# One row of each denominator, laid out by DMA for the reciprocal, and one copy for an even head

## The chip, the cores and the metric

The kernel runs on one core of one Trainium2 chip. The metric is the device time of one execution in microseconds (us). The engines have these names here: TensorE (PE, its weight loads PEld), VectorE (DVE), ScalarE (ACT), GpSimd (POOL) and SyncE (SP), which issues most DMAs.

## What is computed

Three layers follow one another in float32: an attention with a hash mask, a feed-forward layer with the maximum of three products, and one with ELU. The change is in the attention, 16 heads (2 x 8) of 768 positions and 64 columns:

```python
mask = q_bucket[:, :, :, None] == k_bucket[:, :, None, :]
scores = scale * np.matmul(q, k.transpose(0, 1, 3, 2))
scores = np.where(mask, scores, -1000000000.0)
scores = scores - np.max(scores, axis=-1, keepdims=True)
attn = np.exp(scores)
attn = attn / (np.sum(attn, axis=-1, keepdims=True) + 1e-09)
return np.matmul(attn, v).astype(np.float32)
```

The division by the sum of a row is done last, on the outcome of the product with the values.

## The kernel before

The kernel holds its five instruction streams by hand, with semaphores between them. The attention stage runs through slots, from -3 to 18 (`FIRST_SLOT`, `LAST_SLOT`), each of 12 steps; every engine has a function `emit(s)` that is called for each slot and issues in this order whatever that slot has for it. Slot s makes the scores of head s: in each step two products of 128x384 (lines 684, 685) into one of three banks, and ScalarE makes two exponentials of them, `probs` and its rounded `p_hi` (lines 403, 404). GpSimd subtracts the two for `p_lo` (line 336). Six steps later (`LAG`) TensorE multiplies them with the values (lines 699 to 701) into one bank, `pv_ps`. A head has two halves of 384 query positions. Half 0 of head s is finished at the end of slot s, half 1 in the middle of slot s + 1 (line 708 is the last product of either). Meanwhile TensorE multiplies for the row maxima of the next head (line 670, reduced by VectorE at line 540). In odd slots it also transposes the q and k of a coming pair (line 642, at steps 0 and 6, until slot 11), and in even slots it hashes them (lines 654 to 656, at steps 3 and 6, until slot 12).

**The outcome.** `v_hi` has 128 columns: 64 of the head's values and 64 of ones. So the bank has the outcome in partitions 0 to 63 and the denominator of each query in partitions 64 to 127, 64 times the same row. `outcome(s, half)` (line 350), called on ScalarE at steps 0 and 6 ahead of the exponentials, copies both out, each 64x384: the outcome to `x` (line 357), the denominators to `inv` (line 358), in the partitions 0 to 63 for an even head and 64 to 127 for an odd one. A pair of heads fills one unit of 128x384 for each half; four units of `x` and `inv` are in turn. TensorE can start the next half (line 699) when `o_read` says that both copies are done.

**The division.** VectorE takes the reciprocal of a whole unit in two parts of 128x192 (`reciprocals`, line 592), one ahead of maximum 9 of slot u + 2 (`INV_AT`) and one at its end, and multiplies (`divide`, line 587) at the end of that slot. ScalarE rounds the unit to `xh` (line 442) at step 3 of slot u + 3 and GpSimd makes `xl` (line 342) from the rest. The first products of the feed-forward layer read `xh` and `xl`: `piece` in slots 15 and 16 and the experts behind slot 16. A barrier of all engines stands between the attention and the rest.

**SyncE's queue.** In each slot it loads the values of the next head (line 256, behind `vl_done` and `vsum_done`). In even slots it loads the next q and k (`load_qk`, line 230), and then spreads the hashed pair: operands (lines 239, 280), and the bits behind a wait for `bits_done` (line 293). Ahead of slot 12's spread it loads six weight tiles (line 262). Odd slots have nothing but the load of the values, so that the queue runs ahead into the next even slot. In slot 14 ScalarE rounds a weight tile of 128x1536 at step 9 (line 428).

Of the kernel before, what the change touches and what calls it, by code (L numbers as in the profile page):

```python
# [28 lines left out]
FP32 = mybir.dt.float32  # L29
# [8 lines left out]
HEADS = B * H  # L38
# [30 lines left out]
INV_AT = 9  # L69
V_AT, X_AT = 0, 3  # L70
EMPTY_AT = 4


class Slot:
# [17 lines left out]
    has_unit = property(lambda s: 0 <= s.off - 2 < HEADS)  # L92
    has_split = property(lambda s: 0 <= s.off - 3 < HEADS)
    has_tp = property(lambda s: s.odd and -3 <= s.off < HEADS - 3)
# [9 lines left out]
def wait(eng, sem, count):  # L104

    if count > 0:
        eng.wait_ge(sem, count)


def attention(nc, q, k, v, proj, w1, w2, w3, xh, xl, raw, wh, wl, banks, w_loaded, w_split, w_ready, f_ready):  # L110
    ctx = ExitStack()
    with ctx:
# [3 lines left out]
        def sem(name):  # L116
            return ctx.enter_context(nc.semaphore(name))
# [47 lines left out]
        inv = sb("inv", [P, 4, HALF])  # L165

        st_ps = [banks[:, i, :] for i in range(RING)]
        mx_ps = [banks[:, RING + i, :] for i in range(2)]
# [42 lines left out]
        o_read = sem("o_read")  # L211
        inv_done = sem("inv_done")
        x_done = sem("x_done")
        xh_done = sem("xh_done")
# [9 lines left out]
        def _(sp):  # L224
# [23 lines left out]
            load_qk(1, 1, 0)  # L248

            def emit(s):  # L250
                if s.has_max:
# [7 lines left out]
                if s.off == HEADS - 4:  # L259
                    for m in range(2):  # L260
                        for j, w in enumerate((w1, w2, w3)):
                            sp.dma_start(raw[:, m, j * DM:(j + 1) * DM].rearrange("p (t n) -> p t n", n=P),
                                         w[:, m * P:(m + 1) * P].rearrange("(t p) n -> p t n", p=P)
                                         ).then_inc(w_loaded[m], 16)
                if not s.odd and 0 <= s.off < HEADS - 4:

                    load_qk(s.count(0.5, 2), s.off // 2 % 2, s.count(1, 2))
                if s.has_hash:
# [18 lines left out]
                    if s.off == FIRST_SLOT + 3:  # L287
                        sp.wait_ge(consts, 14)
                    both = s.count(1, 4)
                    sp.wait_ge(bits_done, both)  # L290
# [9 lines left out]
        def _(pool):  # L300
# [29 lines left out]
            def emit(s):  # L330
                for step in range(STEPS):
                    if s.has_st:

                        pool.wait_ge(exp_done, s.count(STEPS, step + 1))
                        at = (STEPS * s.off + step) % KEPT
                        pool.tensor_tensor(p_lo[:, at, :], probs[:, step % RING, :], p_hi[:, at, :].bitcast(FP32),  # L336
                                           ALU.subtract).then_inc(pl_done, 1)
                    if s.has_split and step == X_AT:

                        pool.wait_ge(xh_done, s.count(1, -2))  # L340
                        out = bass.ds(s.count(HALF, -3 * HALF), HALF)
                        pool.tensor_tensor(xl[:, out], x[:, (s.off - 3) % 4, :], xh[:, out].bitcast(FP32),
                                           ALU.subtract).then_inc(xl_done, 1)
# [4 lines left out]
        def _(act):  # L348

            def outcome(s, half):  # L350

                h = s.off - 1
                rows, unit = slice(h % 2 * D, h % 2 * D + D), h // 2 * 2 % 4 + half
                if h % 2 == 0 and half == 0:
                    wait(act, xl_done, s.count(1, -3))
                act.wait_ge(pv_ready, s.count(2, half - 1))
                act.activation(x[rows, unit, :], pv_ps[0:D, 0:HALF], ACT.Copy).then_inc(o_read, 1)
                act.activation(inv[rows, unit, :], pv_ps[D:P, 0:HALF], ACT.Copy).then_inc(o_read, 1)  # L358
# [29 lines left out]
            def emit(s):  # L388
                for step in range(STEPS):
# [39 lines left out]
                    if s.has_st and step == EMPTY_AT:  # L429
# [3 lines left out]
                        if s.off == 0:  # L433
# [5 lines left out]
                                       ).then_inc(empty_done, 1)  # L439
                    if s.has_split and step == X_AT:  # L440
                        act.wait_ge(x_done, s.count(1, -2))
                        act.activation(xh[:, bass.ds(s.count(HALF, -3 * HALF), HALF)], x[:, (s.off - 3) % 4, :],
                                       ACT.Copy).then_inc(xh_done, 1)

# [3 lines left out]
        def _(dve):  # L448
# [67 lines left out]
            def emit(s):  # L516
                m = s.off + 1
                for n in range(STEPS):
# [4 lines left out]
                    if n == MAX_BEFORE[V_AT + 2] and s.has_st:  # L523
# [3 lines left out]
                                          v_hi[:, par, :, 0:D].bitcast(FP32), ALU.subtract).then_inc(vl_done, 1)  # L527
                    if n == INV_AT and s.has_unit:
                        reciprocals(s, 1)

                    if n == MAX_BEFORE[TP_AT[0] + 3] and s.has_tp and s.off != FIRST_SLOT + 2:
# [10 lines left out]
                if s.has_max:  # L542
# [3 lines left out]
                                      ).then_inc(max_done, 1)  # L546
                if s.has_unit:
                    reciprocals(s, 0)
# [26 lines left out]
                if s.has_max:  # L575
                    value_sum(s)
                if s.has_unit:
                    divide(s)
                if s.off == HEADS - 2:
# [6 lines left out]

            def divide(s):
                dve.wait_ge(inv_done, s.count(2, -2))
                unit = (s.off - 2) % 4
                dve.tensor_tensor(x[:, unit, :], x[:, unit, :], inv[:, unit, :], ALU.mult).then_inc(x_done, 1)  # L590
# [606 lines left out]
```

## Time and profile before

| | |
|---|---|
| median of three runs | 746.25 us (744.72 to 748.39) |
| the profiled execution | 746.78 us, span 745.0 us |
| TensorE (PE) busy | 721.2 us, 97% of the span |
| ScalarE (ACT) busy | 423.2 us, 57% |
| VectorE (DVE) busy | 383.4 us, 51% |
| GpSimd (POOL) busy | 369.5 us, 50% |
| line 540, maxima, DVE x192 | 99.5 us, 548 ns each |
| lines 403 and 404, exponentials, ACT x384 | 190.1 us, 495 ns each |
| line 336, p_lo, POOL x192 | 198.8 us, 1053 ns each |

The attention stage is the part up to about 297 us. In the page's forty slices of 18.6 us the three other engines are at 7 to 9 tenths there and TensorE at 9:

```profile
PE   6899999999999999999999999999999999999998
...
DVE  6768988989888863322222211244344333444333
ACT  4388989989899882131222121265556555555553
POOL 5277889888888882011110010254544445454442
```

Each digit is the busy share of a slice in tenths. A matmul is pipelined, and its record is longer than the distance to the next one's start; so a TensorE that is shown as busy can still lose time between two starts, which the timeline shows.

### The profile page before, as it was taken

The numbers are of one execution on the slowest core, as the hardware profiler recorded it, in microseconds if no ns is written. First come the engines' busy times: TensorE is split into PE (matmuls) and PEld (weight loads), VectorE is DVE, ScalarE is ACT, GpSimd is POOL, SyncE is SP. The second block draws the span as 40 slices with busy tenths as digits, with TensorE's granted clock in tenths as the row PEclk, the third lists the DMA queues.
The fourth block names the chain that finished last, engine by engine and source line by source line (L and its number), as shares of the span: only waits on it lengthen the run. The fifth ranks groups of instructions, "written<-read, shape, count | busy, mean of one in ns | idle before, by whom it ended". The sixth has DMA issues, their size and how long they took to land.

```text
span 745.0 us, 9831 instructions
## 1 busy us (share of the span) xinstructions
PE 721.2 (97%) x3469; PEld 619.2 (83%) x3469; DVE 383.4 (51%) x616; ACT 423.2 (57%) x820; POOL 369.5 (50%) x333
## 2 busy tenths in 40 slices
PE   6899999999999999999999999999999999999998
PEld 5699998999998877788888888878888888888886
DVE  6768988989888863322222211244344333444333
ACT  4388989989899882131222121265556555555553
POOL 5277889888888882011110010254544445454442
PEclk8799999999999999999999999999999999999999
DMA  7655366563673000311000001133334333443231
GB/s 148 139 129 131 83 134 137 115 131 79 135 181 72 1 0 1 86 42 43 22 21 1 22 22 43 45 103 108 86 111 144 100 98 90 109 141 109 90 99 57
DMA packets 79321, 63.50 MB, mean 85 GB/s; under 512 B 29080, under 2 KB 68712, under 8 KB 79272
## 3 DMA queue, kind: packets, MB, share of 16 engines
q1 hardware_dynamic: 77416, 62.47, 32.8%
q10 hardware_dynamic: 1856, 0.40, 0.3%
q8 instruction: 28, 0.46, 0.3%
q14 instruction: 21, 0.17, 0.1%
HBM read 40.91 MB, written 3.15 MB: 59 GB/s over the span
## 4 chain that ended last, share of the span: by engine, by line
PE 59%; DVE 0%; ACT 0%; issue 0%; DVEq 0%
PE banks L786 14%; PE banks L788 14%; PE banks L787 14%; PE banks L1142 6%; PE banks L1138 6%; PE banks L1139 6%; DVE g_sb L1081 0%; DVE g_sb L1077 0%; DVE e L1061 0%; DVE e L1057 0%; DVE out_sb L1051 0%; ACT gh L1036 0%; ACT neg L1031 0%; ACT e L1008 0%; DVEq L1060 0%
## 5 line engine op out<-in xcount | busy, mean ns | idle before, releaser
L948 POOL TENSOR_TENSOR wl<-raw,wh 128x512 fp32r<-128x512 f32 (+2 forms) x104 | 143.5, 1398 | 296.8 <-ACT wh L964 296.8
L336 POOL TENSOR_TENSOR p_lo<-probs,p_hi 128x384 fp32r<-128x384 f32 x192 | 198.8, 1053 | 55.2 <-ACT p_hi L404 54.3
L786 PE MATMUL banks<-xh,wh 128*128 128x512 f32 x408 | 159.1, 390 | 2.8 <-DVE e L1061 2.6
L787 PE MATMUL banks<-xl,wh 128*128 128x512 f32 x408 | 158.8, 389 | 0.0
L788 PE MATMUL banks<-xh,wl 128*128 128x512 f32 x408 | 158.8, 389 | 0.0
L540 DVE TENSOR_REDUCE half_max<-banks 128x1 f32<-128x384 f32 x192 | 99.5, 548 | 29.0 <-PE banks L670 28.0
L403 ACT ACTIVATE probs<-banks 128x384 f32<-128x384 f32 x192 | 95.0, 495 | 29.2 <-PE banks L685 23.9
L404 ACT ACTIVATE p_hi<-banks 128x384 fp32r<-128x384 f32 x192 | 95.1, 495 | 0.0
L1077 DVE TENSOR_SCALAR g_sb<-banks 128x512 f32<-128x512 f32 x48 | 33.2, 692 | 119.8 <-ACT neg L1031 119.8
L786 PEld LDWEIGHTS banks<-xh,wh 128*128 128x128 f32 x408 | 76.6, 188 | 19.3 <-issue 3.0
L788 PEld LDWEIGHTS banks<-xh,wl 128*128 128x128 f32 x408 | 76.6, 188 | 16.0
L787 PEld LDWEIGHTS banks<-xl,wh 128*128 128x128 f32 x408 | 76.6, 188 | 15.4
L1138 PE MATMUL banks<-wh,gh 128*128 128x512 f32 x192 | 74.9, 390 | 0.2 <-ACT gh L1036 0.2
L1142 PE MATMUL banks<-wh,gl 128*128 128x512 f32 x192 | 74.9, 390 | 0.0
L1139 PE MATMUL banks<-wl,gh 128*128 128x512 f32 x192 | 74.7, 389 | 0.0
L699 PE MATMUL banks<-p_hi,v_hi 128*128 128x384 f32 x192 | 66.8, 348 | 5.9 <-ACT inv L358 5.5
L1031 ACT ACTIVATE neg<-banks 128x512 f32<-128x512 f32 x48 | 28.7, 598 | 68.5 <-PE banks L788 68.5
L964 ACT ACTIVATE wh<-raw 128x512 fp32r<-128x512 f32 (+2 forms) x104 | 64.6, 665 | 2.3
L701 PE MATMUL banks<-p_hi,v_lo 128*64 128x384 f32 x192 | 65.2, 339 | 0.0
L700 PE MATMUL banks<-p_lo,v_hi 128*128 128x384 f32 x192 | 64.4, 335 | 0.0
L1010 ACT ACTIVATE hh<-e 128x512 fp32r<-128x512 f32 x18 | 11.4, 632 | 92.2 <-DVE e L1061 92.2
L1036 ACT ACTIVATE gh<-g_sb 128x512 fp32r<-128x512 f32 x48 | 30.4, 633 | 40.8 <-DVE g_sb L1081 40.8
(121 smaller groups left out, 1191.9 us busy)
## 6 DMA issues: line engine op xcount, KB each, us to landing
operands<-wh SPq DMA_DIRECT2D x36, 384.0 KB, 7.0
raw<-in_moe_w_in SPq DMA_DIRECT2D x48, 256.0 KB, 2.7
raw<-in_moe_w_out SPq DMA_DIRECT2D x48, 256.0 KB, 2.7
raw<-in_moe_w SPq DMA_DIRECT2D x18, 256.0 KB, 3.8
wl<-wh SPq DMA_DIRECT2D x9, 384.0 KB, 6.4
v_raw<-in_v SPq DMA_DIRECT2D x16, 192.0 KB, 2.5
out_dram<-out_sb SPq DMA_DIRECT2D x12, 256.0 KB, 2.1
q_raw<-in_q SPq DMA_DIRECT2D x15, 192.0 KB, 3.6
```

What stands on the lines that cost most here:

```text
L336: pool.tensor_tensor(p_lo[:, at, :], probs[:, step % RING, :], p_hi[:, at, :].bitcast(FP32), ALU.subtract).then_inc(pl_done, 1)
L403: act.activation(probs[:, step % RING, :], scores, ACT.Exp, scale=SCALE)
L404: act.activation(p_hi[:, (STEPS * s.off + step) % KEPT, :], scores, ACT.Exp, scale=SCALE).then_inc(exp_done, 1)
L540: dve.tensor_reduce(half_max[:, m % 2, n // 2, n % 2:n % 2 + 1], bank[:, 0:HALF], AX.X, ALU.max).then_inc(mx_read, 1)
L699: pe.matmul(out, v_hi[:, h % 2, kt, :], p_hi[:, kept, :], start=(kt == 0), stop=False)
L786: pe.matmul(out, sh, mh, start=first, stop=False)
L787: pe.matmul(out, sh, ml, start=False, stop=False)
L788: last = pe.matmul(out, sl, mh, start=False, stop=final)
L948: pool.tensor_tensor(wl[:, j, at:at + cols], raw[:, j, at:at + cols], wh[:, j, at:at + cols].bitcast(FP32), ALU.subtract).then_inc(w_ready, 1)
L1138: pe.matmul(acc[t], gh[:, n % 2, cols], w2h, start=(k == 0), stop=False)
L1139: pe.matmul(acc[t], gh[:, n % 2, cols], w2l, start=False, stop=False)
L1142: last = pe.matmul(acc[t], gl[:, n % 2, cols], w2h, start=False, stop=(k == M2 - 1))
```

## The change

Heads 14 and 15 stay as they are. For heads 0 to 13:

- An even head's outcome and denominators are copied from the bank to `x` in one instruction of 128 partitions, 64 of which the odd head overwrites later. An odd head's are copied in two: the outcome (64x384) as before, and one row of denominators (1x384) to row 64 of `inv`.
- When both halves of a head are out, SyncE gathers its row of 768 denominators into 12 rows of 64 (`rec`, `gather`). ScalarE waits for the even head's gather before it overwrites the rows.
- VectorE takes one reciprocal of 24x64 for each pair (`compact_recips`), ahead of maximum 2 of odd slots. SyncE writes it to DRAM, waits, and broadcasts each head's row of 768 to 64 partitions of `inv` (`spread_recips`).
- The products follow one slot later for the first unit of a pair: both wait for the broadcasts, one at the end of an odd slot, one ahead of maximum 3 of the even slot behind it. The splits into `xh` and `xl` of a pair are both in the even slot, at steps 3 and 9 (3 and 4 in slot 16), and none in odd slots up to 15.

```diff
@@ SyncE
+            def gather(s):
+                h, u = s.off - 1, (s.off - 1) // 2 * 2 % 4
+                a, par = h % 2, h // 2 % 2
+                sp.wait_ge(o_read, s.count(4))
+                sp.dma_start(rec[a * PIECES:(a + 1) * PIECES, par, :], (inv if a else x)[D:D + 1, u:u + 2, :]
+                             ).then_inc(den_in[a], 16)
+            def spread_recips(s):
+                g = (s.off - 3) // 2
+                par, u = g % 2, 2 * g % 4
+                sp.wait_ge(rec_done, g + 1)
+                sp.dma_start(rec_rows[par], rec[:, par, :]).then_inc(rec_out, 16)
+                sp.wait_ge(rec_out, 16 * (g + 1))
+                for a in range(2):
+                    row = rec_rows[par][a * PIECES:(a + 1) * PIECES].rearrange("c n -> (c n)")
+                    sp.dma_start(inv[a * D:(a + 1) * D, u:u + 2, :].rearrange("p a n -> p (a n)"),
+                                 row.unsqueeze(0).to_broadcast([D, S])).then_inc(inv_in, 16)
...
+                if s.has_recip:
+                    spread_recips(s)
+                if s.has_gather and not s.has_hash:
+                    gather(s)
                 if not s.odd and 0 <= s.off < HEADS - 4:
                     load_qk(s.count(0.5, 2), s.off // 2 % 2, s.count(1, 2))
...
+                    if s.has_gather:
+                        gather(s)
                     both = s.count(1, 4)
                     sp.wait_ge(bits_done, both)
@@ ScalarE, outcome
-                if h % 2 == 0 and half == 0:
-                    wait(act, xl_done, s.count(1, -3))
+                if h % 2 == 0:
+                    wait(act, xl_done, s.count(1, half - 4))
                 act.wait_ge(pv_ready, s.count(2, half - 1))
+                if h < HEADS - 2 and h % 2 == 0:
+                    act.activation(x[:, unit, :], pv_ps[:, 0:HALF], ACT.Copy).then_inc(o_read, 2)
+                    return
+                if h < HEADS - 2:
+                    act.wait_ge(den_in[0], 8 * s.off)
+                    act.activation(x[rows, unit, :], pv_ps[0:D, 0:HALF], ACT.Copy).then_inc(o_read, 1)
+                    act.activation(inv[D:D + 1, unit, :], pv_ps[D:D + 1, 0:HALF], ACT.Copy).then_inc(o_read, 1)
+                    return
@@ ScalarE and GpSimd, the splits
+SPLIT_AT = {(HEADS + 1, 3): HEADS - 2, (HEADS + 2, 3): HEADS - 1}
+for g in range(PAIRS - 1):
+    SPLIT_AT[2 * g + 4, 3] = 2 * g
+    SPLIT_AT[2 * g + 4, 9 if 2 * g + 4 < HEADS else 4] = 2 * g + 1
@@ VectorE
-                    if n == INV_AT and s.has_unit:
+                    if n == INV_AT and s.is_direct:
                         reciprocals(s, 1)
+                    if n == 2 and s.has_recip:
+                        compact_recips(s)
+                    if n == 3 and not s.odd and 4 <= s.off <= HEADS:
+                        wait_spread(s)
+                        divide(s.off - 3)
...
-                if s.has_unit:
-                    divide(s)
+                if s.has_recip:
+                    wait_spread(s)
+                    divide(s.off - 3)
+                if s.is_direct:
+                    dve.wait_ge(inv_done, 2 * (s.off - HEADS + 1))
+                    divide(s.off - 2)
...
+            def compact_recips(s):
+                g = (s.off - 3) // 2
+                for a in range(2):
+                    dve.wait_ge(den_in[a], 16 * (g + 1))
+                dve.reciprocal(rec[:, g % 2, :], rec[:, g % 2, :]).then_inc(rec_done, 1)
+            def wait_spread(s):
+                dve.wait_ge(inv_in, 32 * ((s.off - 3) // 2 + 1))
```

`is_direct` holds in slots 16 and 17, `has_gather` in slots 1 to 14, and `has_recip` in the odd slots 3 to 15.

## Rows read from the trace of the kernel before

**Rows 1.** Waits over the whole span: engine line <- awaited: us total, times, longest.
```profile
PEld banks L699 <- ACT inv L358: 11.7, 18, 1.3
...
PE banks L699 <- ACT inv L358: 5.5, 13, 1.0
```

**Rows 2.** Windows: stretch, length, busy time (x instructions) per engine, PEclk, DMA share, GB/s.
```profile
137.90:153.00 15.10, 15.00 (x91) 14.09 (x90) 13.43 (x23) 14.81 (x35) 13.18 (x14) 1.00 0.36 80
122.00:137.90 15.90, 15.58 (x90) 14.58 (x89) 13.92 (x25) 13.79 (x31) 13.17 (x14) 1.00 0.72 158
```

**Rows 3.** Timeline of PE, 145 to 155: start, length, line, operation [idle before].
```profile
145.50 0.34 PE L708 MATMUL banks<-empty,total 128*128 128x384 f32 x1
...
147.22 0.34 PE L685 MATMUL banks<-operands 128*128 128x384 f32 x1
147.66 0.45 PE L699 MATMUL banks<-p_hi,v_hi 128*128 128x384 f32 x1
147.94 0.34 PE L700 MATMUL banks<-p_lo,v_hi 128*128 128x384 f32 x1
148.11 0.34 PE L701 MATMUL banks<-p_hi,v_lo 128*64 128x384 f32 x1
...
154.54 0.44 PE L699 MATMUL banks<-p_hi,v_hi 128*128 128x384 f32 x1 [0.31 <-ACT inv L358]
```

**Rows 4.** Timeline of ACT in the same stretch.
```profile
144.90 0.94 ACT L436 ACTIVATE empty<-operands,below_one 12x768 fp32r<-12x768 f32 x1
...
146.61 0.48 ACT L357 ACTIVATE x<-banks 64x384 f32<-64x384 f32 x1
147.12 0.49 ACT L358 ACTIVATE inv<-banks 64x384 f32<-64x384 f32 x1
```

**Rows 5.** Groups by line, VectorE's reciprocals: busy us, mean ns, idle before.
```profile
L597 DVE RECIPROCAL inv<-inv 128x192 f32<-128x192 f32 x32 | 42.6, 1339 | 9.5 <-ACT inv L358 9.5
```

**Rows 6.** Timeline of ACT, then PE, where slot 6 becomes slot 7.
```profile
137.02 0.49 ACT L404 ACTIVATE p_hi<-banks 128x384 fp32r<-128x384 f32 x1
...
137.93 0.34 PE L684 MATMUL banks<-operands 128*128 128x384 f32 x1
```

**Rows 7.** Timeline of PE in slots 13 to 15, one window, timeline of ACT.
```profile
232.68 0.44 PE L699 MATMUL banks<-p_hi,v_hi 128*128 128x384 f32 x1 [0.18 <-ACT inv L358]
...
240.71 0.44 PE L699 MATMUL banks<-p_hi,v_hi 128*128 128x384 f32 x1 [0.68 <-ACT inv L358]
...
263.73 0.44 PE L699 MATMUL banks<-p_hi,v_hi 128*128 128x384 f32 x1 [1.01 <-ACT inv L358]
...
264.00:268.00 4.00, 4.00 (x16) 3.72 (x16) 2.98 (x3) 3.03 (x9) 4.00 (x5) 0.58 0.00 0
...
251.54 0.53 ACT L442 ACTIVATE xh<-x 128x384 fp32r<-128x384 f32 x1
251.95 0.49 ACT L403 ACTIVATE probs<-banks 128x384 f32<-128x384 f32 x1
...
259.81 1.49 ACT L428 ACTIVATE wh<-raw 128x1536 fp32r<-128x1536 f32 x1
```

**Rows 8.** Timeline of SyncE's DMA issues (merged where xN, N over 1).
```profile
142.08 1.31 SPq L230 DMA_DIRECT2D q_raw<-in_q  x2
...
153.12 1.17 SPq L280 DMA_DIRECT2D operands<-wh  x2
...
204.31 4.17 SPq L262 DMA_DIRECT2D raw<-in_moe_w  x6
```

**Rows 9.** Timeline of DVE, the product at the end of slot 7.
```profile
153.73 0.55 DVE L590 TENSOR_TENSOR x<-x,inv 128x384 f32<-128x384 f32 x1
```

**Rows 10.** DMA issues by line: count, KB each, median us from issue to landing.
```profile
operands<-wh SPq DMA_DIRECT2D x36, 384.0 KB, 7.0
...
v_raw<-in_v SPq DMA_DIRECT2D x16, 192.0 KB, 2.5
...
proj_raw<-in_proj SPq DMA_DIRECT2D x2, 3.0 KB, 4.4
```

More of the change, by code:

```diff
@@ L69 @@
 INV_AT = 9
-V_AT, X_AT = 0, 3
+V_AT = 0
+PIECE = 64
+PIECES = S // PIECE
+SPLIT_AT = {(HEADS + 1, 3): HEADS - 2, (HEADS + 2, 3): HEADS - 1}
+for g in range(PAIRS - 1):
+    SPLIT_AT[2 * g + 4, 3] = 2 * g
+    SPLIT_AT[2 * g + 4, 9 if 2 * g + 4 < HEADS else 4] = 2 * g + 1
 EMPTY_AT = 4
@@ L92 @@
     has_unit = property(lambda s: 0 <= s.off - 2 < HEADS)
-    has_split = property(lambda s: 0 <= s.off - 3 < HEADS)
+    is_direct = property(lambda s: s.has_unit and s.off >= HEADS)
+    has_gather = property(lambda s: 0 <= s.off - 1 < HEADS - 2)
+    has_recip = property(lambda s: s.odd and 3 <= s.off < HEADS)
     has_tp = property(lambda s: s.odd and -3 <= s.off < HEADS - 3)
@@ L165, in attention @@
         inv = sb("inv", [P, 4, HALF])
+        rec = sb("rec", [2 * PIECES, 2, PIECE])
+        rec_rows = nc.dram_tensor("rec_rows", (2, 2 * PIECES, PIECE), FP32, kind="Internal").ap()
         st_ps = [banks[:, i, :] for i in range(RING)]
@@ L212, in attention @@
         inv_done = sem("inv_done")
+        den_in = [sem(f"den_in{a}") for a in range(2)]
+        rec_done = sem("rec_done")
+        rec_out = sem("rec_out")
+        inv_in = sem("inv_in")
         x_done = sem("x_done")
@@ L337, in emit @@
                                            ALU.subtract).then_inc(pl_done, 1)
[L338 to L342, printed above, removed]
+                    if (s.off, step) in SPLIT_AT:
+                        u = SPLIT_AT[s.off, step]
+                        pool.wait_ge(xh_done, u + 1)
+                        out = slice(u * HALF, (u + 1) * HALF)
+                        pool.tensor_tensor(xl[:, out], x[:, u % 4, :], xh[:, out].bitcast(FP32),
                                            ALU.subtract).then_inc(xl_done, 1)
@@ L439, in emit @@
                                        ).then_inc(empty_done, 1)
[L440 to L443, printed above, removed]
+                    if (s.off, step) in SPLIT_AT:
+                        u = SPLIT_AT[s.off, step]
+                        act.wait_ge(x_done, u + 1)
+                        act.activation(xh[:, u * HALF:(u + 1) * HALF], x[:, u % 4, :], ACT.Copy).then_inc(xh_done, 1)
             all_slots(emit)
@@ L576, in emit @@
                     value_sum(s)
-                if s.has_unit:
-                    divide(s)
+                if s.has_recip:
+                    wait_spread(s)
+                    divide(s.off - 3)
+                if s.is_direct:
+                    dve.wait_ge(inv_done, 2 * (s.off - HEADS + 1))
+                    divide(s.off - 2)
                 if s.off == HEADS - 2:
@@ L585, in emit, with divide @@
                                       ).then_inc(w_ready, 1)
-            def divide(s):
-                dve.wait_ge(inv_done, s.count(2, -2))
-                unit = (s.off - 2) % 4
+            def compact_recips(s):
[5 more added lines that the diff above has]
+                dve.wait_ge(inv_in, 32 * ((s.off - 3) // 2 + 1))
+            def divide(u):
+                unit = u % 4
                 dve.tensor_tensor(x[:, unit, :], x[:, unit, :], inv[:, unit, :], ALU.mult).then_inc(x_done, 1)
```

## The prediction

> **What bounds the kernel now.** I read the idle times of the waits view first, then the windows, then the timelines of each engine over two slots. In the attention stage (about 40 to 297 us) TensorE is busy nearly all the time, at the full granted clock: 15.00 of 15.10 us in slot 7 (odd) and 15.58 of 15.90 us in slot 6 (even) [rows 2]. VectorE, at 13.43 and 13.92 us, has a tenth to an eighth of each slot free. So work taken from VectorE is worth nothing unless somebody waits for it. The one wait of TensorE that comes back every slot is line 699, the first product with the values after a half is finished: it waits for ScalarE's second copy out of the bank (line 358), 13 times as idle of the matmuls and 18 times as idle of the weight loads [rows 1]. What those stalls cost is read from starts. Two matmuls of 384 columns start 0.17 to 0.175 us apart (147.94, 148.11) although each record is 0.34 long. Between 147.22 and 147.66 lie 0.44 us, so 0.26 are lost though the row names no idle, and the stalled matmul itself is followed 0.28 instead of 0.17 later: another 0.11 [rows 3]. Where the row shows idle, the loss is that idle plus 0.17, which the record of the matmul before hides, plus the same 0.11: 0.31 in the row at 154.54 is a loss of 0.59 in all.
>
> Why the wait is there differs by slot. In slot 7 the half ends at 145.84, but ScalarE comes to the copies only at 146.61: it has worked without a pause since the slot began (14.81 of 15.10 us), with the empty-row product of 0.94 just before, and two copies in a row then keep the bank until 147.61 [rows 2 to 4]. At the start of an even slot ScalarE is on time, and the two copies (1.0 us) are simply longer than the matmuls in between.
>
> **What the change does to TensorE's stalls.** Heads 0 to 12, the even ones, get one copy of 128 partitions instead of two of 64. The price of one copy goes by the columns: 0.48 for 64x384 and 0.49 for the 128x384 of line 403 [rows 4, 7], so I take 0.49 and the bank is free 0.5 us sooner. Odd slots also lose the split of line 442, 0.41 us from start to the next start [rows 7], and so ScalarE is no longer 0.75 late at 146.61. The even heads' stalls lie in the middle of odd slots and at the start of odd slots (covered by the six transposes there, except in slot 13, which has none).
> Gains: slots 3, 5, 7, 9 and 11, five stalls like that of slot 7, from 0.26 to 0.33 plus about 0.11: 5 x 0.39 = 1.95. Slot 1, where ScalarE has no backlog: 0.22. Slot 13, middle: idle 0.68, loss 0.68 + 0.17 + 0.11 = 0.96. Slot 13, start: idle 0.18, loss 0.46 [rows 7]. Sum 3.6 us. That is the ceiling: the odd heads (stalls of 0.59 at the start of slots 2, 4 and so on, and the middle of slot 14) keep two copies, since a copy of one row has as many columns as one of 64 rows. Between nothing (0.1) and the nearest row (0.49) for the one-row copy I take 0.49; the low end would give 7 x 0.4 = 2.8 us more, and I leave a part of that in the range.
> Costs: the split moves into step 9 of even slots. ScalarE's pass of step 10 of slot 6 ends at 137.51 and the scores of slot 7 that need it start at 137.93: 0.42 of room [rows 6] for an insertion of 0.41. So between 0 and 0.1 in each of slots 4, 6, 8 and 10; I take 0.05, 0.2 in all. In slot 12 nothing covers the next copy, so 0.37 of the 0.46 above comes back. In slot 14 the split stands right behind the 1.49 us of line 428, ahead of the worst stall of the stage (idle 1.01, at 263.73) [rows 7], and goes on top of it: 0.41 to 0.53, I take 0.45. Net: 3.6 - 0.2 - 0.37 - 0.45 = 2.6 us.
>
> **VectorE and the reciprocals.** Heads 0 to 13 lose 28 reciprocals of 1.339 us, 37.5 us of busy time [rows 5], and get 7 of 24x64. If the price follows the columns each is 1.339 x 64/192 = 0.45; the bounds are nothing and the 1.34 of the whole part. Nobody on TensorE's path waits for them: I cost the saving at nothing. What hides the new compact one is VectorE's free time, over 1 us a slot [rows 2].
>
> **SyncE and the DMAs.** New in every slot is a gather (3 KB, 12 rows of 256 B), issued once both halves of a head are out, at mid-slot; in odd slots also one write of 6 KB to DRAM, a wait for it, and two broadcasts of 192 KB. Prices by the nearest rows: a small strided load lands 4.4 us after its issue, 192 KB after 2.5, and 384 KB in a busy queue after 7.0 [rows 10]. Behind the odd slots' gather SyncE now holds the next v load and the four q/k loads. They go out from 142.08 now [rows 8], and at about 147 to 151 after. They land by about 153, just as the operands' spread begins (153.12 [rows 8]), and are read a slot later. Before slot 12 the six weight loads (204.31, 1.5 MB) go out near 210 and run some 2 us into the spread of slot 12; the hash rows behind it have 1 to 2 us of room. I cost both at nothing; with the cover gone it is 1 to 2 us once.
> ScalarE waits for the even head's gather before it overwrites the rows: issued about 146.5, landed at 151 by the slow price and needed once slot 7's last half is out, just after 153. VectorE waits at the third maximum of odd slots for a gather issued 6 us before, and at the end of odd slots for the broadcasts: with slot 7 starting at 137.9 and three maxima ahead of the end of the reciprocal, I put its end at about 141; the write is issued and landed by 141 + 0.65 + 2.5 (or 4.4), broadcasts issued in 1.3, landed 2.5 (or 4.4) later: 148 (or 152). The product starts at 153.73 [rows 9], the latest moment at which the broadcasts cost nothing. It holds, with 2 to 6 us to spare.
> The Trainium skill (DMA: Bandwidth & Descriptors, "Anatomy of one DMA — SWDGE (gpsimd) path") speaks against this route: about 2 us fixed for each transfer, most of it the receipt of the last byte, "surprisingly long" when the target is HBM. With two transfers in series that is 4 us and the data's time, and the broadcasts would still be there before the product, so the sum would be the same; only its "surprisingly long" would be rival (c), below.
>
> **Tail.** Heads 14 and 15 keep the old way. The stage ends with TensorE's products of the first experts, and units 14 and 15 keep their times, so nothing is gained or lost there.
>
> **The sum.** The profiled execution took 746.78 us (span 745.0, 1.8 outside). 746.78 - 2.6 = 744.2. It lies 0.5 over the median of 746.25, from which the same gain gives 743.7: that is the forecast, 0.35% faster. A difference under about 0.5% can hardly be told from none for this kernel, and so "no difference" is the likeliest verdict.
>
> **Rivals.**
> (a) A new wait takes the stall's place: ScalarE's extra split at step 9 costs TensorE 0.4 in each even slot (its room is only 0.42), and the stall in odd slots ends in a wait for the scores. Gain 3.6 - 4 x 0.4 (slots 4, 6, 8, 10) - 0.8 (slots 12 and 14) = 1.2: 745.1. For it: the room of 0.01. Against: ScalarE is idle for 15.90 - 13.79 = 2.1 us of slot 6 [rows 2].
> (b) The clock. After the stall at 263.73 the granted clock falls to the 1.2 GHz level (mean 0.58 over 264 to 268) [rows 7]: 4 x 0.42 x 2 = 3.4 us at half speed, worth up to 1.7 us. If the shift of a few us moves this away, the time is 743.7 - 1.5 = 742.2; the longer stall in slot 14 speaks rather for a drop that stays. The Trainium skill (TensorE: Matmul & The Clock Gate, "Part 1: The HAM clock gate (the "warmup" mystery)") has the clock released by activity, which the fall behind the idle agrees with.
> (c) Slower: the way through DRAM. It decides when the broadcasts land after the end of the odd slot. If the two broadcasts, 64 reads of one row each, take the 7.0 us of the busy queue and the write 4.4, they land at 141 + 0.65 + 4.4 + 1.3 + 7.0 = 154.4, 0.7 too late, and the maxima behind the product keep TensorE waiting. From there every us more costs 7 us, once for each of the seven pairs. 2 us late: 743.7 + 14 = 758. Against: the queues are nearly empty then (mean DMA share 0.36) [rows 2].
> (d) The one-row copy is cheap or odd slots' lower load helps elsewhere: 741.5.
>
> **Chances.** Forecast 0.48 (own range 742.6 to 745.2), (a) 0.20, (b) 0.12, (c) 0.12, (d) 0.08. Faster by over 0.5% (below 742.5): (b), (d) and a little of the forecast, 0.24. Slower by over 0.5% (above 750): (c), 0.12. Within: 0.64. The range leaves out most of (c) and the far end of (d): 741.0 to 747.5.
>
> **What would show it.** In the profile after: line 699's idle after the copy gone in the middle of odd slots, left at 0.31 at the start of even ones; slots 3 to 11 shorter in pairs by 0.4 us; the compact reciprocal near 0.45; VectorE's idle up by some 30 us with no gain from it; the stall near 262 longer by 0.4. The prediction is wrong if VectorE waits for DMAs at the compact reciprocal or the product, if line 670 waits for the hash rows at slot 13, or if a pair of slots gains over 1 us.

## The result

The changed kernel takes 753.06 us (median of five runs, 751.29 to 755.02) against 746.25 before: a ratio of 1.0091, 95% interval 1.0072 to 1.011. It is 6.8 us slower, where 2.6 us less were forecast, and outside the range of 741.0 to 747.5. The profiled execution took 755.02 us, with a span of 753.2.

The page after: first the busy times, then the slices of TensorE and VectorE.

```profile
span 753.2 us, 9862 instructions
...
PE 722.1 (96%) x3469; PEld 618.2 (82%) x3469; DVE 358.2 (48%) x595; ACT 416.7 (55%) x806; POOL 371.2 (49%) x333
...
PE   7899999999999889899999999999999999999998
...
DVE  6757777777786654322222221143434343443333
```

VectorE has 25 us less to do (383.4 before), TensorE the same (721.2 before). The slices of the attention show TensorE at 8 here and there where it had 9. The windows of slots 6 and 7, which answer to [rows 2] (stretch, length, busy time by engine, granted clock, DMA share, GB/s):

```profile
122.40:139.80 17.40, 15.99 (x92) 14.82 (x90) 13.21 (x23) 13.96 (x33) 13.58 (x14) 1.00 0.73 156
139.80:154.60 14.80, 14.80 (x90) 13.96 (x90) 10.97 (x21) 13.76 (x32) 13.13 (x14) 1.00 0.37 93
```

The odd slot behaves as forecast: 14.80 us long instead of 15.10, TensorE busy to the last tenth. The even slot has grown from 15.90 to 17.40, and TensorE is idle for 1.4 us of it. The waits of the attention stage say for whom (answering [rows 1]; us in total, times, longest):

```profile
PEld banks L743 <- DVE half_max L599: 13.7, 17, 1.4
...
PE banks L743 <- DVE half_max L599: 8.2, 10, 1.1
...
PE banks L772 <- ACT inv L409: 2.9, 8, 0.8
PE banks L772 <- ACT inv L412: 2.7, 3, 1.3
```

The wait for ScalarE's copies: the matmuls' idle for it is 2.9 us at line 409, the odd heads' second copy, and 2.7 at line 412, that of heads 14 and 15, which keep the old copies; none is listed for the even heads' single copy (line 403), whose one stall, in the middle of slot 13, is a loss of 0.39 us read from starts. In its place stands line 743, the product for the row maxima, which waits for VectorE (line 599), 8.2 us in ten waits of the matmuls and more of the weight loads. In the waits view of the kernel before that wait was 1.4 us in all. The timeline of TensorE in slot 6 (start, length, line, idle before) shows one of them:

```profile
126.70 0.34 PE L758 MATMUL banks<-operands 128*128 128x384 f32 x1
128.13 0.44 PE L743 MATMUL banks<-operands 96*128 96x384 f32 x1 [1.09 <-DVE half_max L599]
128.41 0.34 PE L727 MATMUL banks<-wh,proj_hi 128*128 128x384 f32 x1
```

From 126.70 to 128.13 are 1.43 us for a distance of 0.17: 1.26 lost, and 0.11 more behind. VectorE's timeline of the same moment:

```profile
124.97 0.56 DVE L599 TENSOR_REDUCE half_max<-banks 128x1 f32<-128x384 f32 x1 [0.42 <-PE banks L743]
125.45 0.86 DVE L580 TENSOR_TENSOR v_lo<-v_raw,v_hi 128x384 fp32r<-128x384 f32 x1
126.24 1.38 DVE L663 TENSOR_TENSOR x<-x,inv 128x384 f32<-128x384 f32 x1
127.54 1.63 DVE L599 TENSOR_REDUCE half_max<-banks 128x1 f32<-128x384 f32 x3
```

Behind maximum 2 (124.97) stand the values' low part, 0.86 us, and then the moved product `x * inv`, 1.38 us. Only at 127.54 do the next maxima follow. The maxima have two banks between TensorE and VectorE (`mx_ps` in the kernel), and TensorE stops once both wait to be read: here 2.0 us lie between VectorE's maxima (125.53 to 127.54).

The lengths of the slots in TensorE's timelines, in us. A slot is measured from start to start of the last product of half 0 (line 708 before, 781 after), and its first half ends where the last product of half 1 starts:

| slot | before | changed | e1, product at 9 | e4, one copy alone | e6, e4 with GpSimd free |
|---|---|---|---|---|---|
| 5, first half | 7.69 | 7.90 | 7.89 | 8.25 | 7.70 |
| 5, second half | 7.38 | 6.94 | 6.95 | 6.94 | 6.95 |
| 6 | 16.06 | 17.36 | 16.05 | 16.05 | 16.04 |
| 12 | 16.05 | 17.34 | 16.03 | 16.04 | 16.02 |
| 13 | 14.76 | 14.61 | 15.91 | 14.17 | 14.18 |
| 14 | 15.04 | 16.27 | 15.03 | 15.06 | 15.05 |
| 15 | 20.00 | 20.46 | 20.44 | 20.02 | 20.03 |

Slots 7, 9 and 11 are like 5, and 4, 8 and 10 like 6, within 0.06 us. The sum over slots 3 to 14 of "changed" less "before": five even slots 6.52, slot 14 1.23, four odd ones -0.89, slot 3 +0.09, slot 13 -0.15. That is +6.8 us, as much as the medians differ. The two profiled executions are 8.2 us apart; the other 1.4 lie outside these slots, where the granted clock falls at different places. One of these places hides a further cost of the change in slot 15, which is taken up behind e9.

### The profile page after: what moved, and what is told of

It is laid out like the page before. It is cut to its first block, busy times and chain, and to the rows that moved or that the text cites. A ratio compares the mean times of both kernels' runs of the same rounds, so it can differ in the third digit from the quotient of the medians.

```text
span 753.2 us, 9862 instructions
## 1 busy us (share of the span) xinstructions
PE 722.1 (96%) x3469; PEld 618.2 (82%) x3469; DVE 358.2 (48%) x595; ACT 416.7 (55%) x806; POOL 371.2 (49%) x333
## 4 chain that ended last, share of the span: by engine, by line
PE 59%; DVE 0%; ACT 0%; issue 0%; DVEq 0%
PE banks L859 14%; PE banks L860 14%; PE banks L861 14%; PE banks L1211 6%; PE banks L1215 6%; PE banks L1212 6%; DVE g_sb L1154 0%; DVE g_sb L1150 0%; DVE e L1134 0%; DVE e L1130 0%; DVE out_sb L1124 0%; ACT gh L1109 0%; ACT neg L1104 0%; ACT e L1081 0%; DVEq L1133 0%
## 5 line engine op out<-in xcount | busy, mean ns | idle before, releaser
L743 PE MATMUL banks<-operands 96*128 96x384 f32 x144 | 43.7, 354 | 10.2 <-DVE half_max L599 7.9
```

## Experiments

Theory A: VectorE's crowd ahead of maximum 3 of the even slots costs the time. Rival B: the new way of the denominators through DMA and DRAM does.

**e1_product_at_9.** The even slots' product of the changed kernel goes ahead of maximum 9, where the kernel before has a reciprocal.

```diff
-                    if n == 3 and not s.odd and 4 <= s.off <= HEADS:
+                    if n == (9 if s.off < HEADS else 3) and not s.odd and 4 <= s.off <= HEADS:
                         wait_spread(s)
                         divide(s.off - 3)
```

> The changed kernel with one edit: in even slots 4 to 14 the product of a pair's second unit stands ahead of maximum 9 on VectorE instead of ahead of maximum 3, where the low part of the values (0.86 us) stands too. Theory A (VectorE's crowd ahead of maximum 3): in the changed kernel TensorE loses 1.26 + 0.12 us at line 743 in each even slot from 4 to 14, waiting for the maximum behind the two operations. With the product at 9 these go, even slots are 16.0 us instead of 17.35, and the time falls by about 6 x 1.3 = 8 us, to 745, near the kernel before. Rival B (the way through DRAM, or the DMAs added, hold the even slots): the product only waits elsewhere, and the time stays within 2 us of 753.

Measured: 746.98 us, 1.0017 of the kernel before (1.0004 to 1.0029). Slot 6 is 16.05 us again. In the slots the line gives back what theory A expected, 7.8 us over the six even slots, but slot 13 gets 1.3 us longer. So the median comes back by 6.1 us, where 8 were expected. VectorE's timeline in slot 6 of this kernel:

```profile
123.75 0.86 DVE L580 TENSOR_TENSOR v_lo<-v_raw,v_hi 128x384 fp32r<-128x384 f32 x1
124.54 1.64 DVE L599 TENSOR_REDUCE half_max<-banks 128x1 f32<-128x384 f32 x3
...
129.72 0.55 DVE L663 TENSOR_TENSOR x<-x,inv 128x384 f32<-128x384 f32 x1
```

The maxima follow the low part at once (124.54), and the same product takes 0.55 us at its new place instead of 1.38. That difference is taken up behind e6.

The medians leave 1.0 us over the kernel before. Against that kernel, slot 13 has 1.15 us too much (15.91 instead of 14.76) and slot 15 0.4, while slots 5, 7, 9 and 11 are 0.9 us shorter together. TensorE's timeline in slot 13, and SyncE's issues before it:

```profile
229.56 0.34 PE L758 MATMUL banks<-operands 128*128 128x384 f32 x1
231.37 0.62 PE L743 MATMUL banks<-operands 96*128 96x384 f32 x2 [1.47 <-DMA operands<-bits]
...
209.15 3.68 SPq L299 DMA_DIRECT2D raw<-in_moe_w  x6
213.26 1.41 SPq L321 DMA_DIRECT2D operands<-wh  x2
214.71 6.07 SPq L256 DMA_DIRECT2D operands<-wh  x4
```

TensorE waits 1.47 us for the hash rows. The six weight loads went out at 209.15 instead of 204.31 [rows 8], the spread of the operands right behind them from 213.26. In the changed kernel itself this stall is almost hidden (a loss of 0.25 us); its slot 12 is 1.3 us longer, which gives the transfers that time.

**e2_before_extra_product.** The other way round: the kernel before with one more product ahead of maximum 3 in slots 4, 6 to 14.

```diff
+                    if n == 3 and not s.odd and 4 <= s.off < HEADS:
+                        dve.wait_ge(x_done, s.off - 2)
+                        dve.tensor_tensor(scratch[:], x[:, (s.off - 3) % 4, :], inv[:, (s.off - 3) % 4, :], ALU.mult).then_inc(extra, 1)
```

> The kernel before with nothing of the change but one added operation: in even slots 4 to 14 VectorE multiplies a unit once more into a tile that nobody reads, ahead of maximum 3, where the changed kernel has its moved product. Theory A: 6 stalls of about 1.3 us at line 670, +7 to +8 us, 1.010 of the kernel before. Rival B: VectorE has room for it, under +1.5 us.

Measured: 753.62 us, 1.0105 (1.009 to 1.012). Its waits show the changed kernel's wait, with almost its sum (8.2):

```profile
PE banks L675 <- DVE half_max L545: 7.9, 8, 1.1
```

The even slots 4 to 12 are 17.35 us long, slot 14 16.28. One operation at that place makes the loss, without anything else of the change.

**e3_after_no_route.** The changed kernel without `gather`, `spread_recips` and the three waits for them; inv and rec are filled with ones at the start.

> The changed kernel without the way of the denominators: no gather, no write to DRAM, no broadcast, and none of the waits for them; it leaves out that part of the computation (the division is by ones laid down at the start, and by the rows that the copies leave). All operations of the engines stay. Theory A: the time stays at 752 to 753, the stall at line 743 in even slots stays at 1.1 us of idle. Rival B: it falls by 6 to 9 us. A third possibility, that the later loads of q, k and the weights cost something once or twice, would show as 0.5 to 2 us.

Measured: 753.25 us, 1.0104 (1.0085 to 1.0123), the changed kernel's time. The wait stays:

```profile
PE banks L739 <- DVE half_max L594: 8.4, 11, 1.1
```

Rival B falls: the route costs nothing that the time shows. The rows of the changed kernel say why: landing of the broadcasts (count, KB, us from issue), the issues of slot 7, and the two small operations.

```profile
inv<-rec_rows SPq DMA_DIRECT2D x14, 192.0 KB, 3.3
...
142.03 0.33 SPq L280 DMA_DIRECT2D rec_rows<-rec  x1
143.33 1.16 SPq L284 DMA_DIRECT2D inv<-rec_rows  x2
149.02 0.82 SPq L272 DMA_DIRECT2D rec<-x  x1
...
L655 DVE RECIPROCAL rec<-rec 24x64 f32<-24x64 f32 x7 | 3.7, 530 | 0.0
...
L409 ACT ACTIVATE inv<-banks 1x384 f32<-1x384 f32 x14 | 6.7, 482 | 0.3
```

The broadcasts go out at 143.33 and land 3.3 us after their issue, long before the product at the end of the slot; and the wait for the write takes 1.3 us with its issue (142.03 to 143.33), with SyncE's next issue only at 149.02.

**e4_before_one_copy.** The kernel before with the one copy of the even heads and nothing else but a tile of ones for the reciprocals.

```diff
+                if h < HEADS - 2 and h % 2 == 0:
+                    act.wait_ge(inv_set, 1)
+                    act.activation(x[:, unit, :], pv_ps[:, 0:HALF], ACT.Copy).then_inc(o_read, 2)
+                    return
```

> The kernel before with only the one copy of 128 partitions for the even heads 0 to 12; it leaves out that their denominators reach the tile of the reciprocals (they divide by ones laid down at the start). The reciprocals, the products and the splits are where they were. By the prediction's sum this is worth 2.8 to 3.6 us (the stalls of TensorE in the middle of odd slots and at slot 13), ratio 0.995 to 0.996. If the stalls only move (its rival a), the gain is under 1 us.

Measured: 745.55 us, 0.9989 (0.9976 to 1.0003): no gain that can be told from none, where the sum had promised 2.8 to 3.6 us. The table shows where it went. The second half of odd slots gained what was forecast (7.38 to 6.94), but their first half went from 7.69 to 8.25. The kernel before, VectorE (the low part of the values, maxima) and GpSimd at the start of slot 7:

```profile
141.01 0.66 DVE L526 TENSOR_TENSOR v_lo<-v_raw,v_hi 128x384 fp32r<-128x384 f32 x1
...
136.71 3.27 POOL L336 TENSOR_TENSOR p_lo<-probs,p_hi 128x384 fp32r<-128x384 f32 x3 [0.18 <-ACT p_hi L404]
140.24 1.01 POOL L336 TENSOR_TENSOR p_lo<-probs,p_hi 128x384 fp32r<-128x384 f32 x1 [0.26 <-ACT p_hi L404]
141.55 1.01 POOL L336 TENSOR_TENSOR p_lo<-probs,p_hi 128x384 fp32r<-128x384 f32 x1 [0.29 <-ACT p_hi L404]
```

and e4_before_one_copy, the same stretch, with TensorE's stall at the end:

```profile
141.07 1.34 DVE L531 TENSOR_TENSOR v_lo<-v_raw,v_hi 128x384 fp32r<-128x384 f32 x1
142.34 1.01 DVE L545 TENSOR_REDUCE half_max<-banks 128x1 f32<-128x384 f32 x2
...
136.77 5.23 POOL L337 TENSOR_TENSOR p_lo<-probs,p_hi 128x384 fp32r<-128x384 f32 x5 [0.19 <-ACT p_hi L409]
...
142.36 0.34 PE L691 MATMUL banks<-operands 128*128 128x384 f32 x1
142.94 0.44 PE L676 MATMUL banks<-wl 96*128 96x384 f32 x1 [0.23 <-DVE half_max L545]
```

Before, GpSimd has subtracted all that it had by 139.98, does one from 140.24 to 141.25, and has nothing until 141.55. VectorE's low part starts at 141.01, with 0.24 us of that subtraction left, and ends 0.42 us behind it: 0.66 us. In e4_before_one_copy ScalarE is through with the copy half a microsecond sooner and begins its exponentials sooner, and GpSimd has five subtractions without a pause up to 142.00. The low part starts at 141.07, 0.09 us behind the start of the last of them, and ends 0.41 us behind its end: 1.34 us. The maxima behind it are late, and TensorE loses 0.40 us at line 676 (142.36 to 142.94). By these rows the copy's shorter time has closed a pause of GpSimd that VectorE lived on. So theory C: VectorE's operations with two operands in SBUF wait for GpSimd's running one.

Slot 13, for which the sum had 1.42 us, gained only 0.59. In its middle TensorE still waits for the one copy:

```profile
240.41 0.45 PE L705 MATMUL banks<-p_hi,v_hi 128*128 128x384 f32 x1 [0.26 <-ACT x L360]
```

By the prediction's rule for such a row that is a loss of 0.26 + 0.17 + 0.11 = 0.54 us, where the sum had taken the whole 0.96 as gained.

**e6_one_copy_gpsimd_free.** In e4's kernel GpSimd fills the low parts of steps 0 to 2 of odd slots with zeros instead of subtracting.

```diff
+                        if s.odd and step < 3:
+                            pool.memset(p_lo[:, at, :].bitcast(FP32), 0.0).then_inc(pl_done, 1)
+                            continue
```

> The kernel before with the one copy of the even heads (as in e4_before_one_copy, which leaves out that their denominators reach the reciprocals), and in odd slots GpSimd fills the low parts of steps 0 to 2 with zeros instead of subtracting, which leaves those low parts out. In e4_before_one_copy the middle of odd slots gained 0.40 us but their first half lost 0.48, where the values' low part on VectorE takes 1.34 us instead of 0.66 while GpSimd subtracts without a pause. Theory C (the two engines hold each other up at SBUF): with GpSimd out of the way the low part takes 0.66 again, the stall ahead of maximum 5 of 0.39 goes, odd slots are 14.7 instead of 15.18, and the time is 2.5 to 3.5 us below e4_before_one_copy. Rival D (the maxima are late for another reason, such as the copies' earlier end): the low part or the stall stays, and the time too.

Measured: 743.03 us, 0.9956 (0.9942 to 0.997), 2.5 us below e4_before_one_copy. VectorE's low part, then GpSimd:

```profile
139.88 0.55 DVE L534 TENSOR_TENSOR v_lo<-v_raw,v_hi 128x384 fp32r<-128x384 f32 x1
...
138.81 0.42 POOL L338 MEMSET p_lo<- 128x384 f32 x1
139.78 0.42 POOL L338 MEMSET p_lo<- 128x384 f32 x1 [0.55 <-ACT p_hi L412]
141.31 0.42 POOL L338 MEMSET p_lo<- 128x384 f32 x1 [1.11 <-ACT p_hi L412]
```

The low part takes 0.55 us, though a fill of GpSimd (139.78 to 140.20) still runs when it starts; the stall is gone, and slots 3 to 11 (odd) are 14.65 to 14.70 us long. The median is 3.3 us below the kernel before of the same runs (746.34). But slots 1 to 14 of the profile are 2.8 us shorter; that, and not the 3.6 us of the prediction, is what the slots show of the copies' ceiling. The Trainium skill (SBUF — State Buffer, "SBUF: two separate sides") has the rule: VectorE and GpSimd share a pair of ports, an exclusive lock for the whole instruction, and a VectorE operation with two SBUF inputs is held up only by a GpSimd operation that reads SBUF. The traces agree in both cases: 1.34 and 1.38 us beside subtractions, 0.55 beside a fill.

The rule holds for the product's two prices too. GpSimd's subtractions from 126.19 to 129.44 in the changed kernel:

```profile
126.19 3.25 POOL L379 TENSOR_TENSOR p_lo<-probs,p_hi 128x384 fp32r<-128x384 f32 x3 [0.29 <-ACT p_hi L458]
```

The product starts at 126.24, has 0.96 us of the first one ahead of it, and ends 0.42 us behind it: 1.38 us. In e1 none runs at 129.72, and it takes 0.55. So 0.83 of the 1.38 us are waiting for GpSimd. Had the product met a free GpSimd ahead of maximum 3, TensorE would have lost about 1.37 - 0.83 = 0.5 us a slot there. That is an estimate from these rows; no run has the one without the other.

**e5_three_moves.** The changed kernel with the product at 9; the split of unit 11 at step 3 of slot 15 instead of step 9 of slot 14; and the six weight loads behind the hash rows of slot 12.

```diff
-    SPLIT_AT[2 * g + 4, 9 if 2 * g + 4 < HEADS else 4] = 2 * g + 1
+    SPLIT_AT[(15, 3) if g == 5 else (2 * g + 4, 9 if 2 * g + 4 < HEADS else 4)] = 2 * g + 1
...
```

> The changed kernel with three moves: the even slots' product ahead of maximum 9 (as in e1_product_at_9); the split of unit 11 at step 3 of slot 15 instead of step 9 of slot 14, where it stands behind line 428's tile; and the six weight loads behind the hash rows of slot 12 instead of ahead of its spread. By the theory the last two take 1.64 us (slot 13's first maximum waited 1.47 for the hash rows in e1_product_at_9) and 0.4 to 1.9 us (the stalls around slot 15's start) off its 747.0: 743.5 to 745. If the weight loads and the split are not what caused those stalls, it stays at 747.

Measured: 747.13 us, 1.0005 (0.9992 to 1.0018), about 2 us over what was expected. Both named stalls are gone or smaller: slot 13 is 14.59 us long, and the stall for the exponentials where slot 14 becomes slot 15 is back from 1.08 to 0.68 us. But a stall stands in the middle of slot 15. TensorE, ScalarE, GpSimd and VectorE there:

```profile
270.18 0.40 PE L861 MATMUL banks<-xh,wl 128*128 128x512 f32 x1
272.48 0.45 PE L772 MATMUL banks<-p_hi,v_hi 128*128 128x384 f32 x1 [1.90 <-ACT inv L412]
...
271.44 0.48 ACT L411 ACTIVATE x<-banks 64x384 f32<-64x384 f32 x1 [2.06 <-POOL xl L386]
...
261.20 9.26 POOL L379 TENSOR_TENSOR p_lo<-probs,p_hi 128x384 fp32r<-128x384 f32 x6 [1.24 <-ACT p_hi L458]
...
265.31 1.78 DVE L614 CAST wh<-raw 128x1536 fp32r<-128x1536 f32 x1
267.12 2.46 DVE L616 TENSOR_TENSOR wl<-raw,wh 128x1536 fp32r<-128x1536 f32 x1
```

TensorE loses 2.07 us for ScalarE's copies, and these wait for GpSimd, which is late. Its six subtractions take 9.26 us. The last two of them stand beside VectorE's large operations on the weight tile (265.31 to 269.58) and take 1.73 and 2.53 us; the second ends 0.87 us behind VectorE's subtraction. Alone one takes 1.01.

The changed kernel has this stall already, in the middle of its slot 15:

```profile
279.43 0.45 PE L772 MATMUL banks<-p_hi,v_hi 128*128 128x384 f32 x1 [1.33 <-ACT inv L412]
```

The second half of its slot 15 is 11.20 us long, against 9.59 before. The move of the split took 0.39 us from the first half and added 0.59 to the second, since ScalarE's copy now waits for the `xl` of unit 11 (line 386), which stands behind those subtractions. In e1's profile the stall doesn't show (second half 9.64): there the granted clock falls to the 1.2 GHz level in the first half, which takes 10.80 us, and TensorE comes to the same place later.

**e7_three_moves_reciprocals.** The same with 21 of the 28 removed reciprocals put back on a tile that nobody reads.

> e5_three_moves with 21 reciprocals of 128x192 put back on VectorE, on a tile that nobody reads, at the places where the kernel before has them (ahead of maximum 9 of odd slots, at the end of slots 2 to 15), 28 us of busy time. By the prediction's step that VectorE's saving is worth nothing: within 0.5 us of e5_three_moves. Rival: the later maxima make TensorE wait, +2 us or more.

Measured: 745.67 us, 0.9991 (0.9979 to 1.0002), 1.5 us below e5_three_moves, where 0.5 either way was expected. In slots 2 to 14 the two agree within 0.25 us each; slot 15 is 19.14 instead of 20.65, since two reciprocals stand there ahead of the large operations and delay them. So taking the reciprocals away is worth nothing in slots 2 to 14, as forecast, and in slot 15 it costs 1.5 us, because it brings the large operations forward into GpSimd's subtractions.

**e8_three_moves_v_later.** e5_three_moves with the low part of the values of odd slots one maximum later, and that of q and k ahead of maximum 7.

> e5_three_moves with the values' low part of odd slots one maximum later (ahead of maximum 4) and the low part of q and k of odd slots ahead of maximum 7 instead of 5, so that fewer operations of two inputs stand in a row ahead of maxima 3 to 5. By theory C odd slots lose about 0.2 us there in e5_three_moves (7.89 instead of 7.70 to their middle): up to 1.2 us less in all, 743 to 744. If the reorder only shifts the stall to maximum 7: no change.

Measured: 745.93 us, 0.9996 (0.9984 to 1.0007). The first half of odd slots falls from 7.90 to 7.82, but the second half rises from 6.95 to 7.19, with a stall ahead of the transposes: odd slots are 15.0 us instead of 14.85. The reorder shifts the stall and makes it larger. Slots 3 and 13 get shorter by 0.25 and 0.47, and slots 3 to 14 come out equal (0.05 us less). The median is 1.2 us lower all the same; nothing in these slots accounts for it, and its cause stays open.

**e9_weights_after_total** and **e10_before_weights_after_total.** The two large operations of slot 15 behind the sum of the values at its end, in e5's kernel and in the kernel before.

```diff
+                if s.has_st:
+                    value_total(s)
                 if s.off == HEADS - 1:
...
                     dve.tensor_tensor(wl[:, 1, :], raw[:, 1, :], wh[:, 1, :].bitcast(FP32), ALU.subtract
                                       ).then_inc(w_ready, 1)
-                if s.has_st:
-                    value_total(s)
```

> e5_three_moves with VectorE's two operations on the weight tile of 128x1536 in slot 15 (a copy of 1.6 to 1.8 us and a subtraction of 2.45 us) behind the sum of the values at the end of that slot instead of ahead of it. In e5_three_moves TensorE lost 2.07 us in the middle of slot 15, waiting for ScalarE's copies, which stood behind GpSimd's subtractions of 1.2 us each; with the 21 reciprocals put back, which delayed those two operations, it lost 0.57. Theory C (GpSimd is held up by VectorE's large operations): slot 15 takes 18.5 to 19.2 us instead of 20.65, the time falls by 1.5 to 2 us against e5_three_moves. Rival: GpSimd is late by its own queue; no change.

> The kernel before with the same single move (the two operations on the weight tile behind the sum of the values in slot 15). It tells whether that gain belongs to the change. The kernel before has in slot 15 the drop of the granted clock and 20.0 us: between no change and 1.5 us less. The change itself, mended, is then the difference between e9_weights_after_total and this: about 1 us (five odd slots 0.22 us shorter), ratio 0.9985.

Measured: e9_weights_after_total 744.2 us, 0.9972 (0.9955 to 0.9988), and e10_before_weights_after_total 745.68 us, 1.0001 (0.9989 to 1.0013). GpSimd in slot 15 of the first:

```profile
261.75 7.02 POOL L379 TENSOR_TENSOR p_lo<-probs,p_hi 128x384 fp32r<-128x384 f32 x6 [1.25 <-ACT p_hi L458]
```

Six subtractions in 7.02 us instead of 9.26: the last two take 1.01 each again instead of 1.73 and 2.53. (The expectation has 1.2 us each for e5; the row gives 1.54 on average.) The kernel is the fastest of this study that computes everything. Slot 15, by halves, in the profiles:

| slot 15 | clock falls in it | first half | second half | whole |
|---|---|---|---|---|
| before | yes | 10.41 | 9.59 | 20.00 |
| e2, before with the extra product | no | 8.86 | 9.62 | 18.48 |
| e10, before with the move | no | 8.85 | 9.62 | 18.47 |
| changed | no | 9.26 | 11.20 | 20.46 |
| e1, product at 9 | yes | 10.80 | 9.64 | 20.44 |
| e5, three moves | no | 8.86 | 11.79 | 20.65 |
| e7, with 21 reciprocals | no | 8.86 | 10.28 | 19.14 |
| e9, e5 with the move | no | 8.86 | 9.57 | 18.43 |

The move is worth 2.2 us in e5's kernel (1.5 to 2 were expected; the medians differ by 2.9, those of the kernel before in the same runs by 0.3) and nothing in the kernel before: e10's slot 15 is 1.5 us shorter than that of the kernel before only because the granted clock doesn't fall in it, and e2 has the same 18.48 us without the move. So the stall in the middle of slot 15 belongs to the change, which took the reciprocals away from ahead of the large operations. In the profiles without the fall slot 15 costs 2.0 us more than before (20.46 against 18.48). With the fall, e1's slot 15 is 0.4 us longer than that of the kernel before.

The mended change is e9 against e10: 744.2 against 745.68 us, 1.5 us less, where about 1 was expected. The profiles' slots 5 to 13 (odd) give 1.1 of it, and slot 3 of e9's takes 0.6 back, most of it in a wait for hash rows at its start. The rest of the 1.5 us is not to be seen in slots 3 to 15.

## Why the prediction was wrong

- **The missing term.** The part on the change lists the reciprocals that VectorE loses and the compact one that it gets, and finds "VectorE's free time, over 1 us a slot". It never costs the product that the change moves from the end of a slot ahead of maximum 3 of the even slots, though the section on the change says so. It is a move of an operation of 0.55 to 1.38 us next to another of 0.86, on the engine that hands TensorE its banks back two at a time. VectorE's free time is a mean over a slot; at that place there was none. This is the step that failed. Price: 6 x 1.3 = 7.8 us (e1, e2), of which the table gives 6.5 for slots 4 to 12 and 1.2 for slot 14. The product at the end of an odd slot is the one that the prediction does cost, and its broadcasts were in time, as it says.
- **The wrong slow rival.** Rival (c) put the loss on the way through DRAM. It had the right sign but the wrong mechanism: e3 shows no change without the route. The broadcasts landed in 3.3 us, within the 2.5 to 4.4 that the forecast took and far from the rival's 7.0; the write with the wait for it took 1.3 us, where 0.65 and 2.5 or 4.4 were taken. The 2 us for each transfer that the prediction quotes from the Trainium skill (DMA: Bandwidth & Descriptors, "Anatomy of one DMA — SWDGE (gpsimd) path") stand there for DMAs that GpSimd issues; this write, which SyncE issued, shows less.
- **The gain.** That the stalls behind even heads' copies would go was right in slots 5 to 11: 0.40 us in the second half of odd slots against 0.39. But the sum has no term for what an earlier copy does to GpSimd and VectorE: 0.17 to 0.5 us came back in the first half, because VectorE's low part met more of GpSimd's subtractions (e4, e6). In the changed kernel the net is 0.22 for an odd slot instead of 0.39. Slot 13 was mis-sized too: 1.42 us taken, 0.59 measured in e4, because TensorE still waits there for the one copy. Without the six products the change gains 0.9 us over slots 3 to 14, against 2.6 forecast.
- **What held.** The extra split at step 9 costs slots 4 to 12 nothing (second halves 7.29 to 7.34 before, 7.31 to 7.34 after), so rival (a) falls. Behind line 428 it added 0.40 us to the stall for the exponentials, against 0.45. The one-row copy takes 0.48 us, as many columns as before, so (d) falls. The compact reciprocal took 0.53 instead of 0.45. VectorE's saving is worth nothing in slots 2 to 14 (e7); that it costs in slot 15 was not foreseen. The late weight loads make a stall of 1.64 us once when the cover is gone (e1), against "1 to 2".
- **The clock.** The fall of [rows 7] is absent from slot 15 after. Instead the granted clock falls to the 1.2 GHz level once in slot 1 (44.8 to 48 us), behind a wait for the hash rows of 1.9 us, and once behind the barrier, where TensorE has been idle for 2.6 us: the mean of 306 to 312 us is 0.72. So (b) gave nothing back. Where the fall stands changes from profile to profile: it costs 1.5 to 1.6 us in the first half of slot 15 (10.41 with it, 8.86 without), and the time from the end of slot 15 to the end of the span is 464.1 us without it and 465.4 to 465.7 with it. The same 2.6 us of idle stand in e9's profile, where nothing falls. A difference of 1 to 1.5 us between two medians is therefore weak evidence here, and the slots' lengths are the better one.

## What to carry to other kernels

When an operation moves, cost it at the place where it arrives, by what stands beside it in that engine's queue, by what the engine next door runs at that moment, and by how many buffers the next engine has until it stops; an engine's mean free time says nothing of that. A copy that ends earlier also starts everything behind it earlier, and can close the very pause that another engine's operation used. And an operation's price is not one number: where the durations of one line spread in the profile, look at which other engine's operation ends a fixed time ahead of the slow ones. Last, an operation that is taken away brings forward what stands behind it, and that too has to be costed where it arrives.

## What the runs showed of the hardware

VectorE's subtraction or product of two SBUF operands (128x384) takes 0.55 us where no subtraction of GpSimd runs at its start (e1, 129.72) and beside a fill (e6, 139.88). Where one already runs, it ends 0.41 to 0.42 us behind that one's end (and never takes less than 0.54), so that its duration goes by what is left: 0.66 with 0.24 left (before, 141.01), 0.87 with 0.45 (before, 156.02), 1.34 with 0.92 (e4, 141.07), 1.38 with 0.96 (changed, 126.24).

The other way round, GpSimd's subtraction of 1.01 us takes 1.73 us beside VectorE's copy of 128x1536 and 2.53 beside its subtraction of 128x1536, and the latter ends 0.87 us behind VectorE's (e5, slot 15). The copy has one operand. The reciprocals of the kernel before, with one operand too, took 1.29 to 1.35 us, and all 32 stood beside subtractions of GpSimd.
